# Layer two of a fused scan and two-layer feed-forward kernel: the piecewise quadratic of one half of the hidden units made with a ramp and its square on ScalarE instead of a clip on VectorE and a biased square on ScalarE

## What is computed

```python
h = x @ w_in                       # layer two, 6080 x 2048
neg = h <= -1.0
pos = h >= 1.0
g = np.where(pos, h, np.where(neg, 0.0, (h + 1.0) ** 2 / 4.0))
out = g @ w_out                    # 6080 x 256
```

## Time and profile before

| | us |
|---|---|
| median of three runs | 1010.28 (1010.21 to 1010.63) |
| the profiled execution | 1009.56 |
| its span in the profile | 1007.4 |

### The profile page before, as it was taken

One profiled execution on the slowest core, in us unless ns is written; L12 is line 12 of the kernel. 1 busy time (PEld: TensorE's weight loads), 2 busy tenths in 40 slices (PEclk: granted clock), 3 DMA queues, 4 the chain that ended last, 5 costly groups with the idle time before them and its releaser, 6 DMA issues.

```text
span 1007.4 us, 11857 instructions
## 1 busy us (share of the span) xinstructions
PE 995.4 (99%) x4387; PEld 823.5 (82%) x4387; DVE 751.4 (75%) x775; ACT 733.7 (73%) x1015; POOL 173.7 (17%) x179
## 2 busy tenths in 40 slices
PE   8999999999999999999999999999999999999997
PEld 6988788888888888888888878878888887888886
DVE  4667578777777766855578788887888878878786
ACT  5766776767867777766776777787787778678764
POOL 2403144422432310001101101200110110110000
PEclk7999999999999999999999999999999999999999
DMA  7534233244244150054430011110200201110112
GB/s 199 109 71 80 63 94 89 106 98 120 110 103 109 41 152 1 1 178 151 144 119 36 1 42 22 21 43 1 42 15 28 43 0 40 25 18 1 22 21 39
DMA packets 160605, 65.45 MB, mean 65 GB/s; under 512 B 142754, under 2 KB 150052, under 8 KB 160548
## 3 DMA queue, kind: packets, MB, share of 16 engines
q1 hardware_dynamic: 152516, 48.02, 20.1%
q0 software_dynamic: 3584, 15.73, 4.2%
q10 hardware_dynamic: 4448, 0.95, 0.5%
HBM read 40.70 MB, written 23.99 MB: 64 GB/s over the span
## 4 chain that ended last, share of the span: by engine, by line
PE 96%; DVE 1%; ACT 1%; DMA 1%; issue 0%; SPq 0%; DVEq 0%; ACTq 0%
PE S L1099 50%; PE U L1083 41%; PE U L1050 4%; DMA extra<-in_f_logit_dram 1%; PE S L1126 1%; ACT keep L571 0%; DVE VF L845 0%; PE S L1035 0%; DVE H L871 0%; DVE H L884 0%; ACT G L620 0%; DVE V L762 0%; DVE V L756 0%; DVE H L863 0%; DVE G L889 0%
## 5 line engine op out<-in xcount | busy, mean ns | idle before, releaser
L1099 PE MATMUL S<-G,W_down 128*128 128x512 f32 (+2 forms) x2280 | 561.2, 388 | 0.1
L1099 PEld LDWEIGHTS S<-G,W_down 128*128 128x128 f32 x2280 | 427.6, 188 | 86.8 <-ACT sent L630 1.5
L1083 PE MATMUL U<-VF,W_up 128*128 128x512 f32 (+1 forms) x1848 | 461.6, 389 | 1.5 <-DVE H L871 1.2
L1083 PEld LDWEIGHTS U<-VF,W_up 128*128 128x128 f32 x1848 | 345.5, 188 | 77.0 <-issue 3.6
L571 ACT ACTIVATE keep<-U 128x512 f32<-128x512 f32 (+1 forms) x352 | 208.9, 594 | 222.2 <-PE U L1083 222.2
L889 DVE TENSOR_TENSOR G<-H,G 128x1024 fp32r<-128x1024 f32 (+3 forms) x208 | 239.1, 1150 | 101.8 <-ACT G L620 101.1
L620 ACT ACTIVATE G<-H 128x1024 fp32r<-128x1024 f32 (+3 forms) x208 | 200.5, 986 | 6.3 <-DVE H L884 3.5
L884 DVE SCALAR_TENSOR_TENSOR H<-H,extra 128x1024 f32<-128x1024 f32 (+1 forms) x96 | 116.0, 1213 | 46.4 <-ACT extra L598 38.4
L871 DVE TENSOR_TENSOR H<-U,keep 128x1024 f32<-128x1024 f32 (+1 forms) x88 | 107.2, 1218 | 49.8 <-ACT keep L571 49.2
L863 DVE TENSOR_TENSOR H<-U,keep 128x1024 f32<-128x1024 f32 (+1 forms) x88 | 106.7, 1213 | 38.0 <-PE U L1083 35.0
L582 ACT ACTIVATE H<-H 128x1024 f32<-128x1024 f32 x80 | 84.3, 1054 | 0.3 <-DVE H L863 0.3
(11 more groups left out here) (80 smaller groups left out, 393.1 us busy)
## 6 DMA issues: line engine op xcount, KB each, us to landing
ready_up<-G POOLq DMA_DIRECT2D x8, 896.0 KB, 3.9
W_up<-ready_up SPq DMA_DIRECT2D x8, 896.0 KB, 6.3
extra<-in_f_logit_dram SPq DMA_DIRECT2D x44, 128.0 KB, 3.3
extra<-in_x_dram SPq DMA_DIRECT2D x44, 128.0 KB, 3.4
middle<-sent SPq DMA_DIRECT2D x22, 256.0 KB, 2.9
V<-middle SPq DMA_DIRECT2D x5, 1024.0 KB, 5.1
out_dram<-extra SPq DMA_DIRECT2D x40, 128.0 KB, 2.8
ready_down<-G POOLq DMA_DIRECT2D x8, 512.0 KB, 2.9
```

What stands on the lines that cost most here:

```text
L1083: mm = nc.tensor.matmul(U[:, bank, 0:w], w_form(j, wp, a), v_form(stage, vp, b), start=fresh and i == 0, stop=i == 2, skip_group_check=True)
L1099: mm = nc.tensor.matmul(S[:, 2 * d + h, 0:w], W_down[:, j, wp, at], g_of(u, e, gp)[:, h * w:(h + 1) * w], start=j == 0 and e == 0 and k == ...
```

## The change

Chunk 1 gets what chunk 0 has. VectorE's `clip` and its semaphore go. ScalarE's `bend` (one activation) becomes `ramp` and `square_ramp` (two), in the same place behind M1 of the next step; `quadratic` uses the minimum for both chunks. The wait for the sum, which the clip had, is now the ramp's. At j = 7 the five low parts stand together, since nothing is between them any more.

```diff
-            def ramp(u):
-                act.wait_ge(s_sum, 2 * (u - PLAIN) + 1)
+            def ramp(u, e):
+                act.wait_ge(s_sum, 2 * (u - PLAIN) + e + 1)
                 if u > SECOND:
-                    act.wait_ge(s_bent, chunk(u - 1 - SECOND, 0))
-                nc.scalar.activation(square_of(u, 0), h_of(u, 0), ACT.Relu, bias=half[:, 0:1], scale=0.5
+                    act.wait_ge(s_bent, chunk(u - 1 - SECOND, e))
+                nc.scalar.activation(square_of(u, e), h_of(u, e), ACT.Relu, bias=half[:, 0:1], scale=0.5
                                      ).then_inc(s_ramp, 1)
...
-            def bend(u):
-                e = 1
-                act.wait_ge(s_clip, u - SECOND + 1)
-                nc.scalar.activation(square_of(u, e), square_of(u, e), ACT.Square, bias=half[:, 0:1], scale=0.5
-                                     ).then_inc(s_square, 1)
+            def square_ramp(u, e):
+                act.wait_ge(s_ramp, chunk(u - SECOND, e))
+                nc.scalar.activation(square_of(u, e), square_of(u, e), ACT.Square).then_inc(s_square, 1)
...
                 elif u - 1 < UNITS:
-                    bend(u - 1)
+                    ramp(u - 1, 1)
+                    square_ramp(u - 1, 1)
...
-            def clip(u):
-                e = 1
-                dve.wait_ge(s_sum, 2 * (u - PLAIN) + 2)
-                if u > SECOND:
-                    dve.wait_ge(s_bent, chunk(u - 1 - SECOND, e))
-                nc.vector.tensor_scalar(square_of(u, e), h_of(u, e), -1.0, 1.0, ALU.max, ALU.min).then_inc(s_clip, 1)
...
-                                               op0=ALU.max, op1=ALU.min if e == 0 else ALU.mult).then_inc(s_bent, 1)
+                                               op0=ALU.max, op1=ALU.min).then_inc(s_bent, 1)
```

More of the change, by code:

```diff
@@ L183, in build @@
         s_sum = sem("s_sum")
-        s_clip = sem("s_clip")
         s_ramp = sem("s_ramp")
@@ L582, in leaky @@
                 nc.scalar.activation(h_of(u, e), h_of(u, e), ACT.Prelu, alpha=0.01).then_inc(s_leaky, 1)
-            def ramp(u):
-                act.wait_ge(s_sum, 2 * (u - PLAIN) + 1)
+            def ramp(u, e):
+                act.wait_ge(s_sum, 2 * (u - PLAIN) + e + 1)
                 if u > SECOND:
-                    act.wait_ge(s_bent, chunk(u - 1 - SECOND, 0))
-                nc.scalar.activation(square_of(u, 0), h_of(u, 0), ACT.Relu, bias=half[:, 0:1], scale=0.5
+                    act.wait_ge(s_bent, chunk(u - 1 - SECOND, e))
+                nc.scalar.activation(square_of(u, e), h_of(u, e), ACT.Relu, bias=half[:, 0:1], scale=0.5
                                      ).then_inc(s_ramp, 1)
-            def square_ramp(u):
-                act.wait_ge(s_ramp, u - SECOND + 1)
-                nc.scalar.activation(square_of(u, 0), square_of(u, 0), ACT.Square).then_inc(s_square, 1)
-            def bend(u):
-                e = 1
-                act.wait_ge(s_clip, u - SECOND + 1)
-                nc.scalar.activation(square_of(u, e), square_of(u, e), ACT.Square, bias=half[:, 0:1], scale=0.5
-                                     ).then_inc(s_square, 1)
+            def square_ramp(u, e):
+                act.wait_ge(s_ramp, chunk(u - SECOND, e))
+                nc.scalar.activation(square_of(u, e), square_of(u, e), ACT.Square).then_inc(s_square, 1)
             def g_high(u, e):
@@ L744, in _ @@
                 if live:
-                    ramp(u)
-                    square_ramp(u)
+                    ramp(u, 0)
+                    square_ramp(u, 0)
             for i in range(4):
@@ L1011, in _ @@
                 if last:
[L1012 to L1017, removed]
+                    for i in range(len(SINGLES)):
                         single_low(ahead, i)
```

## The result

| | before | changed |
|---|---|---|
| median of four runs each, us | 1010.45 (1010.21 to 1012.71) | 1031.76 (1030.71 to 1033.87) |
| the profiled execution, its span | 1009.56, 1007.4 | 1032.24, 1030.4 |

The ratio is 1.0205, with a 95% interval from 1.0188 to 1.0222: 21.3 us slower. Forecast were 1027.7 with a range from 1020 to 1033. The direction and the mechanism came as forecast; about 4 us were missing.

What follows compares the result with a forecast made beforehand. TensorE, 99% busy, was taken to be bound by a loop through ScalarE and VectorE from step start to step start. The terms summed to 17.8 us, taken as 17.4: 1010.28 + 17.4 = 1027.7 us, range 1020 to 1033.

Steps and rivals of the forecast that it cites:

- The loop: Layer two, step start to next: M1 through ScalarE to U2, then VectorE's sum, low part, sum; 10.40 us against 10.20.
- The tie: Between M1 and U2: second high part may start at M1+4.04, ScalarE reaches it at M1+4.06; no addition.
- Ordinary steps: 1024-wide steps of layer two without transposes: each grows by 0.20 us, bounds 0 and 0.31 (with a matmul refill).
- Steps with transposes: Eight 1024-wide steps; transposes between chunk 0's low part and sum no longer fit: +1.05 us each, bounds 0.75 and 1.1.
- Stage ends: j = 7, where VectorE makes the next stage's first low part behind chunk 1's sum: +0.71 us, five times.
- First and second steps: Start of a stage: first steps -0.1 us, five times, as U2 comes slightly earlier; second steps 0.
- 17 x 0.20: Layer two's ordinary 1024-wide steps, j = 2 to 6 of the first stage, j = 2, 5, 6 of four more: 3.4 us.
- Last stage and end: 960-token stage: three ordinary steps at +0.1 us, two with transposes at +0.9; one more activation at the end, +0.8.
- Only transposes and ends: Rival: loop 10.2 us or less, so ordinary steps cost nothing; 11.0 us in all, 1021 us; chance 0.12.
- room enough: Rival: ScalarE's extra 1.1 us a step fits its idle time, so no change, 1010.3 us; chance 0.04.
- faster: Rival: without the clip, waits at stages' second steps go, -2.5 us in all, 1007.8 us; chance 0.03.
- Worse: Rival: product 6 waits for U2 and the second high part for the quadratic, adding 10 us, about 1037; chance 0.09.

Runs made afterwards that it cites:

- copies in the loop: Kernel before, with two copies of 512 and 448 unused columns added on ScalarE behind bend in every step of layer two: 1033.21 us, ratio 1.0224.
- copies behind U2: Kernel before, with the same two copies of unused columns on ScalarE placed behind its copy U2, where ScalarE idles: 1011.09 us, ratio 1.0008.
- U2 early: Changed kernel with ScalarE's copy U2 made between the two high parts instead of behind both: 1024.96 us, ratio 1.0143.

## Why the prediction was right, and where it fell short

- **What bounds the kernel.** The loop was the right object: its two halves were reckoned as 5.01 and 5.39 us and measured as 5.02 and 5.38. The second half rested on the one place where the loop was closed already. The tie that the first half allowed for, second high part against second quadratic, held without an addition. The copies in the loop and behind U2 showed that the place decides: 1033.2 against 1011.1 us for the same work.
- **Ordinary steps.** +0.20 forecast; +0.25 to +0.27 in layer two's first stage and +0.17 to +0.22 later. The bound of 0.31 held. Why the first stage's are the longer ones was not looked into.
- **Steps with transposes.** +1.05 forecast, +0.98 to +1.00 measured. Mis-sized by 0.05 to 0.07: packed, sum, low part and sum follow each other a few hundredths closer than the pitches I took. Cutting and moving the transposes confirmed the term.
- **Stage ends.** +0.71 forecast, +0.68 to +0.73 measured.
- **First and second steps.** -0.5 forecast, -1.1 measured. 0.4 of the difference is one step of 10.86 in the kernel before, the largest of the five there (the copies behind U2 leave that part of the kernel alone, and their trace has 10.51 in its place); the others are -0.10 to -0.15. The clip's removal did reach them, as that run showed (2 us for the clip alone).
- **j = 6, the step that failed.** The term "17 x 0.20" counted five steps as ordinary that are not. The prediction moved VectorE's instruction by a microsecond without asking what GpSimd does at that time; it had GpSimd at nothing without a reason. The trace of before held the hint: GpSimd's pair beside VectorE's low part, stretched to 3.55 us. Measured +5.1 us for the five instead of 1.0, and 4.0 of them go with GpSimd's work cut. That the time still lies in the range, 1.2 us under its upper end, is partly luck: none of the unknowns that the range was made for was this one.
- **Last stage and end.** +2.9 forecast, +3.3 measured. 0.35 of it is one step (j = 6, 10.22 us) in which the sum of chunk 0 starts 0.49 us behind the end of its copy instead of 0.13. GpSimd has no work there. The step is there in the changed kernel, with GpSimd's work cut and with the transposes cut or moved (10.18 to 10.22), but not with the copies in the loop (9.98) or with U2 early (9.77).

```profile
1002.49 1.16 DVE L857 TENSOR_TENSOR H<-U,keep 128x960 f32<-128x960 f32 x1 [0.65 <-ACT keep L570]
```

The step of 10.86 in the kernel before is of the same kind: its sum of chunk 0 starts 0.49 us behind the copy's end too. The cause stays open. One hint, not tried: in all five traces that have the late sum a packet of the instruction queue (`q14 instruction` in the profile's list of DMA) starts some 0.67 us behind the sum's start, and with the copies in the loop there is none in that step. With U2 early there is one 0.46 us behind a sum that is not late, so the hint shows nothing yet.

- **The rivals.** "Only transposes and ends" fell with the ordinary steps; "room enough" with the two runs with copies: behind U2 there is room for the work, between M1 and U2 there is not; "faster" came true in part (first and second steps), as less than what is lost. "Worse" priced the waits for U2 in the middle of a step: they did not come.

## What to carry to other kernels

Where the busiest engine waits now and then for another, find the loop that closes there and add up its parts from starts, not busy shares: a microsecond of work outside it cost next to nothing here (0.8 us in 47 steps), while inside, what goes beyond the slack comes back in every turn. In the changed kernel moving one copy ahead of one activation gave 6.8 us and moving the transposes into a wait 8.1, where the choice of function itself, with these out of the way and GpSimd's two instructions cut, costs some 2. And when instructions shift in time on VectorE, look at what GpSimd runs at the new time: which of the two waits depends on who comes first.

## What the hardware showed that I had not expected

VectorE's low part (two inputs in SBUF, the memory on the chip) takes 1.22 us alone, and 2.03 or 2.31 us when a GpSimd instruction on SBUF has begun before it. It then ends 1.08 us behind GpSimd's end, however early it started. With the order reversed it is GpSimd's instruction that is longer, 2.29 against 1.30 us, and ends 1.17 us behind VectorE's end.

And a loop that is 0.2 us too long hardly shows on TensorE. At an ordinary start of the changed kernel the weight loads wait 0.2 to 0.4 us, the matmuls show no idle time at all, and the first nine of them take 2.28 to 2.37 us instead of 2.20. The step grows by about 0.2, less than the weight load's wait, because that load has 0.22 us of lead to lose. Such a loop is found in the waits of the weight loads and in the distance between starts, not in the matmuls' idle time.
